# Tuned two-stage kernel on one core: last chunks hand on no state, first states are copied by ScalarE, flags are compared at the end, middle slots are written out

## The reference, cut to what matters

```
S_re, S_im = 0                                   # (B, H, D, D)
for t in range(S):
    new_re = ar * S_re - ai * S_im               # ar, ai: normalised decay of token t
    new_im = ar * S_im + ai * S_re
    S_re, S_im = new_re + k_t v_t^T, new_im
    y[:, :, t] = q_t @ S_re
x = y as (3072, 384)
g = softplus(x @ w_in)          # 384 -> 2048
x2 = g @ w_out                  # 2048 -> 384
out = ((x2 @ w1) * (x2 @ w2)) @ w3 @ w_out2      # 384 -> 1024, 1024 -> 384
```

## Time and profile before

| | us |
|---|---|
| median of 3 runs | 1051.46 |
| lowest, highest run | 1050.67, 1052.08 |
| profiled execution | 1052.62 |
| its span | 1050.8 |
| PE busy in the span | 933.9 (89%) |
| DVE busy | 613.4 (58%) |
| ACT busy | 426.8 (41%) |
| granted PE clock, mean | 0.953 |

### The profile page before, as it was taken

How to read it: one execution, slowest core, us unless ns; L and a number is a source line. 1 busy time by engine, 2 the same in 40 slices (tenths; PEclk the granted TensorE clock), 3 DMA queues, 4 the chain that set the end, 5 groups by cost and what they waited for, 6 DMA issues and landing times.

```text
span 1050.8 us, 15307 instructions
## 1 busy us (share of the span) xinstructions
PE 933.9 (89%) x5538; PEld 841.2 (80%) x5538; DVE 613.4 (58%) x997; ACT 426.8 (41%) x602; POOL 70.2 (7%) x56
## 2 busy tenths in 40 slices
PE   0965659989989989989989999999899999999998
PEld 0544559988979979879879899899788888888887
DVE  5977878878879879879888732345221212121211
ACT  3161253663664664654654654478011111111011
POOL 0000000000000000000000000000121212121311
PEclk9985569999999999999989999999899999999999
DMA  9584183480470560560660440042101010101000
GB/s 337 205 219 146 44 197 80 132 198 12 137 192 13 144 184 13 147 182 11 172 160 8 136 107 12 9 166 79 44 1 60 1 60 0 60 0 60 1 31 31
DMA packets 99382, 99.54 MB, mean 95 GB/s; under 512 B 7664, under 2 KB 92656, under 8 KB 99312
## 3 DMA queue, kind: packets, MB, share of 16 engines
q1 hardware_dynamic: 99312, 98.60, 32.8%
HBM read 63.96 MB, written 29.88 MB: 89 GB/s over the span
## 4 chain that ended last, share of the span: by engine, by line
PE 52%; DVE 22%; DVEq 9%; ACT 7%; issue 5%; DMA 3%; SPq 2%; ACTq 0%
PE ps_p L1222 6%; PE ps_p L1223 6%; PE ps_p L1224 6%; DVE sp L1114 3%; PE ps L1222 3%; PE ps L1224 3%; PE ps L1223 3%; DVEq L874 3%; PE ps_ay L1258 3%; PE ps L1404 3%; PE ps L1406 2%; PE ps L1405 2%; DVE ms L872 2%; SPq L404 2%; DVE g_l L1121 2%
## 5 line engine op out<-in xcount | busy, mean ns | idle before, releaser
L1222 PE MATMUL ps<-g_h,wo_h 128*128 128x384 f32 x384 | 134.9, 351 | 6.0 <-DVE g_l L1121 5.3
L615 POOL TENSOR_TENSOR abl<-ab,abh 128x512 fp32r<-128x512 f32 x48 | 69.3, 1444 | 972.2 <-DVE abh L1204 972.2
L1224 PE MATMUL ps<-g_h,wo_l 128*128 128x384 f32 x384 | 129.7, 338 | 0.0
L1223 PE MATMUL ps<-g_l,wo_h 128*128 128x384 f32 x384 | 129.5, 337 | 0.0
L1222 PE MATMUL ps_p<-x1h,win_h 128*128 128x384 f32 x336 | 119.1, 354 | 9.1 <-DVE sp L1114 7.0
L1224 PE MATMUL ps_p<-x1h,win_l 128*128 128x384 f32 x336 | 114.8, 342 | 0.0
L1223 PE MATMUL ps_p<-x1l,win_h 128*128 128x384 f32 x336 | 114.7, 341 | 0.0
L709 ACT ACTIVATE g_h<-sp 128x768 fp32r<-128x768 f32 (+1 forms) x71 | 55.4, 781 | 109.2 <-DVE sp L1114 108.7
L1258 PE MATMUL ps_ay<-stq,stk 96*128 96x128 f32 x384 | 58.4, 300 | 38.7 <-DMA vt<-in_v 12.7
L1195 DVE TENSOR_TENSOR ab<-ps_ay,bc 128x512 f32<-128x512 f32 x24 | 16.6, 693 | 123.8 <-ACT bc L841 123.8
L1258 PEld LDWEIGHTS ps_ay<-stq,stk 96*128 96x128 f32 x384 | 54.3, 212 | 43.0 <-issue 30.2
(11 more groups left out here) (149 smaller groups left out, 2082.9 us busy)
## 6 DMA issues: line engine op xcount, KB each, us to landing
qk_scr<-tt SPq DMA_DIRECT2D x16, 576.0 KB, 5.5
stq<-qk_scr SPq DMA_DIRECT2D x48, 192.0 KB, 4.6
qk_scr<-pp SPq DMA_DIRECT2D x16, 576.0 KB, 4.0
stk<-qk_scr SPq DMA_DIRECT2D x48, 192.0 KB, 4.6
an<-in_a_re SPq DMA_DIRECT2D x8, 576.0 KB, 4.2
an<-in_a_im SPq DMA_DIRECT2D x8, 576.0 KB, 5.2
qk<-in_q SPq DMA_DIRECT2D x8, 576.0 KB, 8.2
qk<-in_k SPq DMA_DIRECT2D x8, 576.0 KB, 9.2
```

The lines of the kernel that those rows point to most:

```text
L615: tensor_tensor(abl[:, m % AR, :], ab[:, m % 2, :], abh[:, m % AR, :].bitcast(F32), ALU.subtract).then_inc(ab_lo, 1)
L1222: mm(o, wh, xh, start=start, stop=False)
L1223: mm(o, wh, xl, start=False, stop=False)
L1224: return mm(o, wl, xh, start=False, stop=stop)
```

## The change

- `hands_on(m, i)` is true for every group of an even tile and for groups 0 to 3 of an odd one. For groups 4 and 5 of an odd tile (the last chunk of a sequence) the four transposes, ScalarE's copy to kt, the z matmuls and DVE's addition are left out. `states(m, i)` gives the new counts that s_new and kt_ev are waited for.
- In an even tile the copy of groups 0 and 1 into the state moves from DVE's new_state to ScalarE, behind the copy of the outputs in y_out.
- The flags: the squares' sums go to columns of their own for each tile, ScalarE copies the last column of the squared product between Ln and Exp of prep_inverse, and DVE's three small operations for each tile go. Behind slot 6 two comparisons over all tiles, a drain and the reduction follow.
- On all engines the loop over slots 1 to 4 is written out, and its waits compare with constants.

```
+        def hands_on(m, i):
+            return m % 2 == 0 or i < 4
+        def states(m, i):
+            return 10 * (m // 2) + NG * (m % 2) + min(i, 4 if m % 2 else NG)
...
-            with eng.Fori(0, 2) as b:
-                slot(2 * b + 1, True, True, True)
-                slot(2 * b + 2, True, True, True)
+            for n in range(1, NT - 3):
+                slot(n, True, True, True)
...
                 act(te[:, 1, :], te[:, 0, :], ACT.Ln)
                 eng.drain()
+                act(stats[:, 5 * m + 2:5 * m + 5].unsqueeze(2), by_g(te[:, 0, :])[:, :, T - 1:T], ACT.Copy).then_inc(end_ev, 1)
                 act(te[:, 1, :], te[:, 1, :], ACT.Exp, scale=-1.0).then_inc(prep_inv, 1)
...
             def k_by_tokens(m, i):
+                if not hands_on(m, i):
+                    return
...
                 act(ys[0:64 + D, i % 2, :, :], ps_y[0:64 + D, 0:HQ // 2, :], ACT.Copy).then_inc(y_ev, 1)
+                if m % 2 == 0 and i < 2:
+                    act(state[:, HQ * i:HQ * i + HQ, :], ps_z0 if first else ps_z, ACT.Copy).then_inc(s_new, 1)
...
-                ve.tensor_scalar(stats[:, 13:15], stats[:, 0:2], SQ_MAX, None, ALU.is_le)
...
-                ve.tensor_scalar(stats[:, 15:18].unsqueeze(2), by_g(te[:, 0, :])[:, :, T - 1:T], P2_MIN, None, ALU.is_ge)
...
-                ve.tensor_tensor(stats[:, 8:13], stats[:, 8:13], stats[:, 13:18], ALU.mult)
...
-            def new_state(m, i, even, z=ps_z):
+            def new_state(m, i, z=ps_z):
+                if not hands_on(m, i) or m % 2 == 0 and i < 2:
+                    return
...
-            ve.tensor_reduce(stats[:, 18:19], stats[:, 8:13], AXX, ALU.min).then_inc(ok_all, 1)
+            eng.wait_ge(end_ev, NT)
+            per_tile = stats[:, 0:5 * NT].rearrange("p (m x) -> p m x", x=5)
+            ve.tensor_scalar(flags[:, :, 0:2], per_tile[:, :, 0:2], SQ_MAX, None, ALU.is_le)
+            ve.tensor_scalar(flags[:, :, 2:5], per_tile[:, :, 2:5], P2_MIN, None, ALU.is_ge)
+            eng.drain()
+            ve.tensor_reduce(stats[:, 5 * NT:5 * NT + 1], flags[:, :, :].rearrange("p m x -> p (m x)"), AXX, ALU.min)\
+                .then_inc(ok_all, 1)
...
-                        eng.wait_ge(s_new, NG * m + i)
+                        eng.wait_ge(s_new, states(m, i))
...
-                for h4 in range(HQ):
+                for h4 in range(HQ if hands_on(m, i) else 0):
                     h = HQ * hq + h4
                     last = nc.tensor.transpose(ps_kt[:, h4, :], stk[0:D2, h, cs], ident[:, :])
...
-                eng.wait_ge(kt_ev, NG * m + i + 1)
-                for h4 in range(HQ):
+                if hands_on(m, i):
+                    eng.wait_ge(kt_ev, states(m, i + 1))
+                for h4 in range(HQ if hands_on(m, i) else 0):
                     h = HQ * hq + h4
                     last = mm(z[:, h4, :], kt[:, i % 2, h4, :], vt[:, c, D * h:D * h + D], start=True, stop=True)
```

More of the change, by code:

```diff
@@ L510, in _ @@
             slot(0, True, True, first=True)
-            with eng.Fori(0, 2) as b:
-                slot(2 * b + 1, True, True)
-                slot(2 * b + 2, True, True)
+            for n in range(1, NT - 3):
+                slot(n, True, True)
             slot(NT - 3, True, True, nxt=False)
@@ L643, in prep_squares @@
                 for i in range(2):
-                    last = act(te[:, i, :], an[:, i, :], ACT.Square, accum_out=stats[:, i:i + 1])
+                    last = act(te[:, i, :], an[:, i, :], ACT.Square, accum_out=stats[:, 5 * m + i:5 * m + i + 1])
                 last.then_inc(prep_sq, 1)
@@ L1067, in mask_scores @@
                                  ALU.mult).then_inc(a_masked, 1)
-            def new_state(m, i, even, z=ps_z):
+            def new_state(m, i, z=ps_z):
+                if not hands_on(m, i) or m % 2 == 0 and i < 2:
+                    return
                 eng.wait_ge(yz_mm, NG * m + i + 1)
                 hs = slice(HQ * (i % 2), HQ * (i % 2) + HQ)
-                if even and i < 2:
-                    ve.tensor_copy(state[:, hs, :], z).then_inc(s_new, 1)
-                else:
-                    ve.tensor_tensor(state[:, hs, :], state[:, hs, :], z, ALU.add).then_inc(s_new, 1)
+                ve.tensor_tensor(state[:, hs, :], state[:, hs, :], z, ALU.add).then_inc(s_new, 1)
             tokens_mask()
@@ L1133, in slot @@
                     if att and 1 <= j <= NG:
-                        new_state(n + 1, j - 1, not even)
+                        new_state(n + 1, j - 1)
                     if has_prep and j < 6:
@@ L1164, in _ @@
             slot(0, True, True, True, True)
-            with eng.Fori(0, 2) as b:
-                slot(2 * b + 1, True, True, True, False)
-                slot(2 * b + 2, True, True, True, True)
+            for n in range(1, NT - 3):
+                slot(n, True, True, True, n % 2 == 0)
             slot(NT - 3, True, True, False, False)
             slot(NT - 2, True, False, False, True)
-            ve.tensor_reduce(stats[:, 18:19], stats[:, 8:13], AXX, ALU.min).then_inc(ok_all, 1)
+            eng.wait_ge(end_ev, NT)
[5 more added lines that the diff above has]
+                .then_inc(ok_all, 1)
             eng.wait_ge(ok_cnt, 1)
@@ L1254, in scores @@
                     else:
-                        eng.wait_ge(s_new, NG * m + i)
+                        eng.wait_ge(s_new, states(m, i))
                 for h4 in range(HQ):
                     h = HQ * hq + h4
-                    mm(ps_a[:, h4, :], stk[0:D2, h, cs], stq[0:D2, h, cs], start=True, stop=True)
-                for h4 in range(HQ):
+                    last = mm(ps_a[:, h4, :], stk[0:D2, h, cs], stq[0:D2, h, cs], start=True, stop=True)
+                for h4 in range(HQ if hands_on(m, i) else 0):
                     h = HQ * hq + h4
@@ L1271, in outputs @@
                 if not fresh:
-                    eng.wait_ge(s_new, NG * m + i - 1)
+                    eng.wait_ge(s_new, states(m, i - 1) if i else states(m, 0) - 1)
                 if first and i:
@@ L1283, in outputs @@
                         h = HQ * hq + 2 * s_ + u
[L1284 to L1287 removed]
+                        last = mm(ps_y[64 * u:64 * u + D, s_, :], vt[:, c, D * h:D * h + D], am[:, i % 2, 2 * s_ + u, :],
+                                  start=fresh, stop=True)
+                if hands_on(m, i):
+                    eng.wait_ge(kt_ev, states(m, i + 1))
+                for h4 in range(HQ if hands_on(m, i) else 0):
                     h = HQ * hq + h4
@@ L1351, in _ @@
             slot(0, True, True)
-            with eng.Fori(0, 2) as b:
-                slot(2 * b + 1, True, False)
-                slot(2 * b + 2, True, True)
+            for n in range(1, NT - 3):
+                slot(n, True, n % 2 == 0)
             slot(NT - 3, True, False)
@@ L1359, in _ @@
             eng.wait_ge(ok_all, 1)
-            eng.wait_ge(s_new, NG * NT)
-            mm(ps_k[0:1, 0:1], stats[:, 18:19], ones[:, 0:1], start=True, stop=True).then_inc(ok_cnt, 1)
+            eng.wait_ge(s_new, states(NT, 0))
+            mm(ps_k[0:1, 0:1], stats[:, 5 * NT:5 * NT + 1], ones[:, 0:1], start=True, stop=True).then_inc(ok_cnt, 1)
             slot(NT - 1, False, False, nxt=False)
@@ L1380, in _ @@
             eng.wait_ge(a_masked, NG * NT)
-            eng.wait_ge(kt_ev, NG * NT)
-            eng.wait_ge(s_new, NG * NT)
+            eng.wait_ge(kt_ev, states(NT, 0))
+            eng.wait_ge(s_new, states(NT, 0))
             def up2(t, u, m):
```

9 lines of the change are left out of this document (4 added, 5 removed).

## The result

| | before | after |
|---|---|---|
| median, us | 1051.46 | 1040.19 |
| lowest to highest of 5 runs, us | 1048.87 to 1052.94 | 1036.74 to 1042.12 |
| profiled execution, us | 1052.62 | 1040.19 |
| its span, us | 1050.8 | 1038.4 |
| PE busy, us | 933.9 (89%) | 920.1 (89%) |

The ratio of the times is 0.9883, with a 95% interval from 0.9858 to 0.9907. The forecast was 1041.2 us, its range 1037.8 to 1045.3. The runs of the changed kernel spread by 5.4 us. Two of the five, 1036.74 and 1036.98, had a mean granted PE clock of 0.960, the other three, 1040.19 to 1042.12, had 0.952 to 0.955: much of the spread goes with PE's clock.

A forecast was written before the change was run, and what follows sets the result against it. DVE sets the fronts; PE, then a chain of ys and its DMA, sets the tails. Terms -7.8 - 1.1 - 1.8 - 0.5 + 0.35 + 0.5 = -10.35 us take 1052.62 to 1042.3, median 1041.2, range 1037.8 to 1045.3.

The forecast's parts named there:

- tails: Stretch from group 4's scores to the next L887, set by PE, then by ys, its DMA, x1h and x1l.
- fronts: Stretch from DVE's L887 to the scores of group 4; DVE sets its length, so PE work saved there counts nothing.
- item 1: Last chunks without keys by tokens and state, in tails of slots 0, 2, 4, 6: 1.95 us each, -7.8 us.
- Item 3: Middle slots written out: four fronts 0.45 us each, -1.8 us; tails and loop's edge -0.5; PE's 1.99 us stall nothing.
- rival B: More low clock: fronts of three or four slots fall for 6.9 us, 1044 to 1046 us; chance 0.10.
- Rival D: Slower: low clock moves into tails, where PE is the bound; with four such stretches 1054.4 us; chance 0.03.
- rival A: DVE keeps the tails: those of slots 0, 2, 4 give only 1.2 us each, 1043.5 us; chance 0.14.
- Item 2: First states copied by ScalarE, in fronts of slots 1, 3, 5: 0.27 us a copy, four count, -1.1 us.
- Rival C: PE's 1.99 us stall is real gain, or slots 1 and 5 lose low clock: 1038 to 1039.5 us; chance 0.12.
- Item 4: Flags: dropping DVE's three small operations gives 0; comparisons, drain and longer reduction at the end cost +0.35 us.
- Item 5: PE's half clock in fronts: slot 3 may fall too, others may be spared; +0.5 us, bounds -2.7 and +3.
- rival E: Fronts swallow everything: only slot 6, the copies and the register waits count, 1047 us; chance 0.05.

The follow-up runs named there:

- f_fill: The changed kernel with 13 or 15 unread matmuls added on PE in step 0 of slots 1 to 5, where it waits: 1036.64 us, ratio 0.9861.
- u_last: The changed kernel with the last chunks' transposes, copies, z matmuls and additions put back: 1047.83 us, ratio 0.9970.
- e_unroll: The kernel before with only the middle slots written out, on all engines: 1048.82 us, ratio 0.9981.
- u_states: The changed kernel with the first states copied by DVE again: 1040.03 us, ratio 0.9897.
- g_flag: The changed kernel with PE doing up(7, 1) ahead of the flag's matmul instead of behind it: 1037.30 us, ratio 0.9865.
- i_split: The changed kernel with two of the five y stores of group 5 issued by ScalarE: 1038.23 us, ratio 0.9869.
- h_both: The changed kernel with both f_fill's extra matmuls and g_flag's up(7, 1) ahead of the flag's matmul: 1033.63 us, ratio 0.9833.
- h_states: h_both with the first states copied by DVE again: 1034.66 us, ratio 0.9834.
- e_unroll_dve: The kernel before with the middle slots written out on DVE alone: 1049.14 us, ratio 0.9978.
- e_unroll_pe: The kernel before with the middle slots written out on PE alone: 1053.00 us, ratio 1.0016.
- h_flags: h_both with DVE's three small flag operations of each tile put back beside the new ones: 1035.30 us, ratio 0.9837.
- j_all: h_both with two of the five y stores of group 5 issued by ScalarE: 1034.56 us, ratio 0.9835.

## Why the forecast came true, and where it did not

The time was right, 1040.19 us against 1041.2 (the sum itself gives 1041.1). The profiled executions differ by 12.4 us where the sum said 10.35, and 1.84 us of that come from the prologue, of which the sum has nothing.

That the remaining 10.6 us lie so near to the forecast is in part luck. By place the forecast holds: tails -8.0 us (forecast -8.3), fronts -2.6 (-2.4), the end +0.34 (+0.35), and -0.44 from slot 5 to 6, where nothing was forecast. But within the tails, item 1 gave 0.8 us and the written-out loop 0.5 us more than forecast, and late stores and transfers took 1.7 us back (the five tails against f_fill's). Within the fronts, the changes gave some 3.7 us instead of 2.9 once the low clock is taken off on both sides, and the clock took 1.1 us instead of 0.5.

Three of the forecast's own signs would have misled. Item 3 was to be wrong if the fronts of slots 2 and 4 stayed at 48.4 us, and slot 2's is 48.58; slot 3's was to fall to 47.4 us and is 48.52. Both have low clock, and without it (f_fill) they are 47.65 and 47.51 us. And low clock in slot 2 was to mean rival B or D, but their times (1044 us and more) did not come.

**Item 1** was forecast at 1.95 us a tail. The runs show 2.13 to 2.16 in slots 0, 2 and 4 and 2.14 in slot 6, 8.6 us against 7.8 and above the forecast's bound of 7.84; the total of u_last bears it out from both sides, 7.6 by the medians and 9 by the ratios. The step was right, its size too small, because a group's matmuls were priced from their own start to the next start. From the scores of group 4 to the first matmul of down it was 350.37 - 349.13 = 1.24 us with the transposes and is 0.89 without, which is 0.35 and not 0.28. From the last L1284 to ys it was 365.02 - 363.79 = 1.23 us with the z matmuls and is 358.76 - 358.33 = 0.43 without, which is 0.80 and not 0.70. With the z matmuls of group 4 read in the same way (0.71) a tail gives 2 x 0.35 + 0.80 + 0.71 = 2.2 us.

The follow-up of that step came out too. PE pauses 0.36 us before down(n, 6), waiting for DVE's g_low, and that costs nothing: with the stores undelayed the pause before up(n + 1, 0) falls from 0.91 us to 0.31. So rival A, DVE keeping the tails, fell. What the forecast didn't have is that the chain from ys on is SP's: five stores take 3.06 us to issue, at times 3.58 or 3.89, and each delay reaches L900 in full. In the profiled run of the changed kernel that made slot 2's tail 26.87 us, above what the forecast asked of it, and slot 3's 28.69. Whether this is the change's cost stays open. Every version has such delays in most slots, and at the stores of group 4 they cost nothing: in e_unroll these take 4.20 us in slot 2 and 3.04 in slot 3, and the tails are 28.20 and 28.21 us. In the tails of slots 0 to 4 it is 0.4 us or more on the stores of group 5 in four profiled executions only, and these are the versions that have item 1 and no filling (the changed kernel, u_states, g_flag, i_split), each in slots 2 and 3.

**Item 2**, 0.27 us a copy: right at 0.28. Without low clock the first copies count too, so six may count and not four; the 1.25 us of slots 0 to 5 between h_both and h_states fall short of six (1.7 us) because h_both alone has pauses of DVE in slots 4 and 5. The other way, 0.2 us of the 1.25 are slot 1's tail in h_states, where SP's stores took 3.27 us. That no gain can be seen when it is undone in the changed kernel (u_states) is the clock's doing.

**Item 3**, 0.45 us a front and nothing for PE's stall: both right, as far as the fronts can be read. DVE alone written out gives 1051.45 - 1049.14 = 2.3 us, all engines 1050.55 - 1048.82 = 1.7, against a forecast of 2.3 with the tails; their intervals overlap. The totals are not clean of the clock: of the 2.5 us that e_unroll_dve's profiled execution gains from slot 0 to 5, 1.24 are slot 5's, whose code is unchanged and whose low clock is 3.4 us long instead of 6.8. In the fronts it is spread unevenly, 0.83 us in slot 2 and 0.27 in slot 4, partly because DVE pauses in slot 2 of before (0.31 us at 328.97) and in slot 4 of e_unroll_dve (0.49 us at 469.56). In slot 1, with 3.4 us of low clock in both, it is 0.38. In slot 3 the low clock hides it. Rival C's first half, that the 1.99 us is real, fell by e_unroll_pe: PE alone written out gave 1.0016. The Trainium skill (Runtime: NRT & Kernel Launch, Instruction fetch mechanics) has it that a taken branch can make an engine wait, and the trace agrees with 1.99 us; its advice to unroll fully gave that back nowhere here, because PE is not what the front waits for. In the tails the loop's edge was right (28.62 or 28.64 to 28.20 in slot 2), though it was not PE's or DVE's alone, and whether it was ScalarE's or SP's was not tried; the five tails together gave 1.0 us, not 0.5. From slot 5 to 6 e_unroll and e_unroll_dve also take 0.4 us less than before (70.87 and 70.86 against 71.25), though these two slots were written out before; that is not explained.

**Item 4**: the end was forecast at +0.35 us and is +0.34. In the fronts the step "next to nothing" was a little wrong: the comparison on 2 numbers costs 0.07 us where it stands (1.51 against 1.44) and the clean front 0.11. Taking the operations away thus saves some 0.5 us in five fronts, within the bound of -0.8, where 0 was taken; h_flags could not show it in a total. The larger thing, which the forecast named as idle time and passed by, was at the same place: PE idles 2.85 us before the flag's matmul, and moving one `up` ahead of it gives 1.9 to 2.9 us (g_flag).

**Item 5**, the clock, was forecast at +0.5 us with bounds from -2.7 to +3, the widest term. Its reasoning held in kind: slot 3 fell once it was written out (in e_unroll_pe and in e_unroll_dve too, though not in u_last and u_states), and slot 5 was spared in the profiled execution. The fill shows that the pauses are needed: with them filled, no slot falls. They are not enough, since slot 5 of the changed kernel has them and did not fall. What could not be forecast is which slots fall: slots 1, 2 and 3 in the changed kernel, 1, 4 and 5 in u_states, 3 and 5 in g_flag, whose code in slots 1 and 2 is the changed kernel's. The price of 1.9 us for 6.8 us of low clock was too small: slot 1's front is 49.52 us with it and 47.13 without, 2.4 us, and 3.4 us of it cost 0.9 to 1.0. By these prices the changed kernel's profiled execution pays 2.4 + 0.9 + 1.0 = 4.3 us in its fronts and before's paid 1.0 for 3.4 us of it in slot 1 and 2.2 for 6.8 us in slot 5 (49.93 against 47.76 in e_unroll, the same code without low clock), so the term is +1.1 and not +0.5. Rival C's second half, the low clock vanishing, happened in slot 5 alone, whose front fell by 2.42 us; rival B, three or more fronts with low clock, happened in slots 1 to 3, with shorter stretches than it asked for.

Not in the forecast at all: 1.84 us came before the scores of slot 0, where the change has next to nothing to take. Over all kernels of this study the mark lies anywhere from 192.56 (j_all) to 195.45 us (h_flags), with no relation to the edits that I can see. The prologue's low clock lasts 78.6 us in all in before and 68.3 in the changed kernel, but 75 us in both h_states (193.28) and h_flags, so it isn't the whole reason. But where it falls goes with the mark: in the two kernels with the earliest marks, the changed one and j_all (192.56), PE has 10.2 us of full clock from 95.7 and 95.5 us on, amid the first tile's groups, and from the scores of group 1 to those of group 5 it takes 19.3 us, in all others 20.6 to 21.6. So most of the 1.84 us went with the clock in the prologue. Why it differs there stays open. Without this stretch the span would have lost 10.6 us against the forecast 10.35. Rival D, low clock in a tail, was seen in no kernel; rival E, the fronts swallowing what the tails give, fell by u_last: the fronts behind the shortened tails are those of slots 1, 3 and 5. With item 1 undone they are 49.55, 47.20 and 47.15 us. Slot 1's, with 6.8 us of low clock in both, is 49.52 in the changed kernel; the other two, at full clock, are 47.51 and 47.49 in f_fill, where DVE pauses in both slots. None grew by the 2 us that came off the tail ahead of it.

## What to carry to other kernels

Ask of each microsecond on a busy engine who waits for it: here PE's work in the tails counted in full and more than its own duration, while a stall of 2 us in the fronts was worth nothing. Where PE's clock at times falls behind a row of short pauses, small gains can't be read until the pauses are filled, be it with matmuls that nobody reads; do that first and measure edits on that base. And look at single points where every engine waits for one small result: work that doesn't depend on it should be ahead of it in the queue.

## What the runs showed of the hardware that was not expected

- PE's granted clock fell to half behind three pauses of 0.91, 1.37 and 0.89 us with matmuls between them, for 3.4 us, and in slot 1 for 6.8; none of them is long alone. The same pauses (0.90, 1.38, 0.89) in slot 5 left it at 1.00.
  The Trainium skill (TensorE: Matmul & The Clock Gate, Part 1) has the array throttled unless its activity releases it; f_fill agrees with it, 1.00 in every slot and 1036.64 us with 71 more matmuls.
- Code without loops has stalls too. DVE shows pauses for which nothing in the trace is the reason, some 0.4 to 0.5 us, at most one a slot (slots 3, 4 and 5 of the changed kernel), such as this one in slot 5 of the changed kernel:

```profile
539.56 0.96 DVE L1129 TENSOR_TENSOR g_l<-sp,g_h 128x768 fp32r<-128x768 f32 x1 [0.49 <-issue]
```

  They move when code is added or taken away: h_both has them at 400.84, 469.51 and 534.78, h_states at 400.15 alone, h_flags and u_last none between 200 and 600 us. A front with one is 47.5 or 48.0 us, without 47.13 or 47.65. What they are was not tried.
- Two DMAs issued by ScalarE hold it for 0.53 and 0.87 us, 1.4 us together in a tail without delay; five issued by SP take 3.06 us. At times one issue takes up to 1.3 us longer, and in i_split, where both engines issue at once, both were held until the same moment (359.49). What holds them was not tried.
- ScalarE's copy of 3 numbers a partition takes 0.21 us, not the up to 0.39 us that the forecast allowed.
